# A hand-ordered attention and expert kernel: the second matrix's products run a whole tile behind the first's

## The reference

```python
def _attn_ref(q, kv, w_sr):                 # B=2, N=12288, C=128; kv is 384 x 32 per batch
    kv_pool = kv.reshape(B, H // 4, 4, W // 4, 4, C).mean(axis=(2, 4))
    k = v = kv_pool.reshape(B, -1, C) @ w_sr            # 768 keys
    a = softmax(q @ k.T / sqrt(C))
    return a @ v

def _moe_ref(x, w_gate, w1, w2):            # E=8 experts, D=128, F=1024
    e = argmax(x @ w_gate); gate = softmax(x @ w_gate)[e]
    return gate * (relu(x @ w1[e]) @ w2[e])

def _moe2_ref(x, w_gate, w_output_gate, w1, w2):
    # as _moe_ref, and the result is also scaled by sigmoid(x @ w_output_gate)[e]
```

## Time and profile before

| what | value |
|---|---|
| time, median of 3 runs | 1875.98 us (1874.28 to 1877.02) |
| span of the profiled execution, first to last instruction | 2009.7 us |
| busy in that span | PE 1918.1, DVE 1342.6, ACT 1054.8, POOL 739.4 us |
| attention stage in the profile | up to about 640 us |
| layer 1's tiles in the profile | about 640 to 1377 us |
| layer 2's tiles in the profile | about 1377 to 1994 us |

### The profile page before, as it was taken

How to read it: one execution, slowest core, us unless ns; L and a number is a source line. 1 busy time by engine, 2 the same in 40 slices (tenths; PEclk the granted TensorE clock), 3 DMA queues, 4 the chain that set the end, 5 groups by cost and what they waited for, 6 DMA issues and landing times. The chain is left out here.

```text
span 2009.7 us, 53289 instructions
## 1 busy us (share of the span) xinstructions
PE 1918.1 (95%) x15716; PEld 1879.5 (94%) x15716; DVE 1342.6 (67%) x3525; ACT 1054.8 (52%) x2333; POOL 739.4 (37%) x823
## 2 busy tenths in 40 slices
PE   9999999999999999998999989899999999999998
PEld 7999999999999989898898889888999999999998
DVE  6788887888887666565566666666655555555555
ACT  3777777777776344344344444343444444444444
POOL 5456643466643323222222222222333333333333
PEclk8999999999999999999999999999999999999999
DMA  8355532355533211111321111142211114141111
GB/s 301 104 169 174 178 102 74 109 172 175 173 114 125 67 49 50 42 46 44 118 92 44 45 48 42 51 135 74 66 44 46 43 42 165 42 163 43 46 44 36
DMA packets 138040, 185.88 MB, mean 92 GB/s; under 512 B 17425, under 2 KB 95380, under 8 KB 134368
## 3 DMA queue, kind: packets, MB, share of 16 engines
q1 hardware_dynamic: 112640, 134.16, 20.9%
q0 software_dynamic: 25312, 50.65, 7.1%
HBM read 98.41 MB, written 87.63 MB: 93 GB/s over the span
## 5 line engine op out<-in xcount | busy, mean ns | idle before, releaser
L1718 DVE SCALAR_TENSOR_TENSOR h_lo<-psum,h_hi 128x512 fp32r<-128x512 f32 x800 | 541.2, 688 | 248.3 <-ACT h_hi L1509 198.4
L1509 ACT ACTIVATE h_hi<-psum 128x512 fp32r<-128x512 f32 x800 | 460.6, 598 | 259.1 <-PE psum L1303 244.9
L1303 PE MATMUL psum<-x_hi,w 128*128 128x256 f32 x1600 | 344.7, 290 | 66.6 <-DVE x_lo L1712 48.7
L413 POOL DMA_INDIRECT y_bucket<-kv_store,place x200 | 194.3, 971 | 542.1 <-DVE place L379 484.5
L1303 PE MATMUL psum<-x_hi,w_split 128*128 128x256 f32 x1600 | 339.6, 287 | 9.2 <-issue 2.8
L997 POOL DMA_INDIRECT out<-rows x200 | 193.9, 970 | 405.0 <-DVE rows L1738 368.5
L1303 PEld LDWEIGHTS psum<-x_hi,w 128*128 128x128 f32 x1600 | 270.2, 192 | 75.5 <-issue 55.2
L1320 PE MATMUL psum<-h_hi,w 128*128 128x256 f32 x1600 | 321.6, 285 | 0.7 <-DVE h_lo L1718 0.7
L413 POOL DMA_INDIRECT x_bucket<-rows,place x192 | 190.0, 990 | 293.2 <-DVE place L379 197.7
L1303 PEld LDWEIGHTS psum<-x_hi,w_split 128*128 128x128 f32 x1600 | 265.5, 189 | 17.4 <-issue 10.5
L1320 PEld LDWEIGHTS psum<-h_hi,w 128*128 128x128 f32 x1600 | 266.4, 195 | 1.3 <-DVE h_lo L1718 1.3
(11 more groups left out here) (177 smaller groups left out, 4385.1 us busy)
## 6 DMA issues: line engine op xcount, KB each, us to landing
w_table<-w_split SPq DMA_DIRECT2D x64, 512.0 KB, 3.5
w_raw<-in_moe_w SPq DMA_DIRECT2D x64, 256.0 KB, 4.1
xr<-x_bucket SPq DMA_DIRECT2D x100, 132.0 KB
xr<-y_bucket SPq DMA_DIRECT2D x100, 132.0 KB
kv_store<-in_kv SPq DMA_DIRECT2D x24, 512.0 KB, 9.3
q_in<-in_q SPq DMA_DIRECT2D x48, 256.0 KB, 2.7
w<-w_table SPq DMA_DIRECT2D x12, 1024.0 KB, 6.8
w_split<-w_table SPq DMA_DIRECT2D x8, 1024.0 KB
```

Of the source, the lines that this page charges most:

```text
L413: nc.gpsimd.indirect_dma_start(r.bucket[:, :], bass.IndirectOffsetOnAxis(r.place[:, g, s:s + 1], 0), r.rows[:, g, s, LG:], None, bounds_ch ...
L1303: ins = nc.tensor.matmul(bank[p][:, m * BLOCK:(m + 1) * BLOCK], layer.w1[c % 2][:, hl, f], x[:, c % 2, :], start=k == 0, stop=k == 2)
L1509: nc.scalar.activation(h_hi[:, p, :], bank[p][:, :], ACT.Relu).then_inc(h_hi_done, 1)
L1718: nc.vector.scalar_tensor_tensor(h_lo[:, p, :], bank[p][:, :], 0.0, h_hi[:, p, :].bitcast(F32), ALU.max, ALU.subtract).then_inc(h_lo_done, 1)
```

## The change

The order inside a tile is written anew on PE, ACT and DVE. On PE it becomes: down 0 of c-1; turn_x of c+1; up 0 of c; down 1 of c-1; rank; up 1; down 2 of c-1; up 2; rows of c-2; down 3 of c-1; up 3. All of `down` runs a tile behind `up`, and the rows and gates' products two tiles behind. `down` alternates between bank 4 and bank 7 by tile, and the routing's small results move from bank 7 to bank 6, which the rows also use; so PE now waits at `ranks` until DVE has read the rows of tile c-3, and at `bank_read` until DVE has read the rank's result. A new small DVE instruction per tile, `keep_tags`, copies the token numbers and gates out of `xr` into `tags`, so SP may refill the slot when that is done. SP asks for x first, then the first matrix of tile c+2, then the second matrix of tile c+1 (before: of tile c+2). The one-time steps of the plan move by one tile.

```diff
-        q_bank, o_bank, rank_bank = bank[5], bank[6], bank[7]
+        q_bank, o_bank = bank[5], bank[6]
+        x_bank, tile_bank = bank[5], bank[6]
+        down_banks = [bank[4], bank[7]]
...
         STEPS = {
             1: ["top", "below", "scaled", "cand", "best", "onehot", "sum", "placed", "den"],
-            2: ["skip", "top", "below", "cand", "best", "onehot", "opened", "open_z", "sum", "eps", "den", "placed"],
+            2: ["skip", "top", "below", "cand", "best", "onehot", "opened", "open_z", "placed", "sum", "eps", "den"],
         }
...
-                    wait(pool, up_done, i - NIT if r.n == 1 else i, HP * UNROLL, HP * (2 * gc + 5) + 2)
+                    wait(pool, up_done, i, HP * UNROLL, HP * (2 * gc + 6) + 2)
...
                     if live(i, c, limit[0], UNROLL):
-                        wait(sp, row_step, i, RS * UNROLL, RS * (c - 3))
+                        wait(sp, tags_done, i, UNROLL, c - 3)
                         load_x(i, c, layer_of(i, c, n)).then_inc(x_in[c % 4], 16)
...
-                        sel = opens(i, c + 2, n)
-                        next_w(i, c + 2, n, sel, 0)
                         next_x(i, c + 3, n)
-                        next_w(i, c + 2, n, sel, 1)
+                        next_w(i, c + 2, n, opens(i, c + 2, n), 0)
+                        next_w(i, c + 1, n, opens(i, c + 1, n), 1)
...
                                 pe.wait_ge(p_lo_done, PAIRS * NBLK)
+                            if at(i, c, 1):
+                                pe.wait_ge(r1.row_step, NBLK)
                             wait(pe, layer.w2_in[c % 2], i, 32, 16 * (c // 2 + 1) - 8 * layer.first)
-                            wait(pe, yT_done, i, UNROLL, c)
+                            wait(pe, yT_done, i, UNROLL, c - 1)
...
+                    if c % 2 and routed(i, n) and live(i, (c - 5) // 2, r2.groups, 2):
+                        rank(pe, r2, i, (c - 5) // 2, True)
+
+                def bank_read(i, c, n):
+
+                    if at(i, c, 0) or at(i, c, 2):
...
+                    if c % 2 and routed(i, n) and live(i, (c - 5) // 2, r2.groups, 2):
+                        ns = len(r2.steps)
+                        wait(pe, r2.route_step, i, 2 * ns, ns * ((c - 5) // 2) + r2.steps.index("placed") + 1)
 
                 def tile_body(i, n):
                     for c in range(UNROLL):
                         if at(i, c, 0):
                             add_pv(NIT, -1, PAIRS - 1, 1)
+                        down(i, c - 1, 0, n)
+                        turn_x(i, c + 1)
                         up(i, c, 0, n)
+                        down(i, c - 1, 1, n)
+                        ranks(i, c, n)
+                        up(i, c, 1, n)
                         down(i, c - 1, 2, n)
+                        up(i, c, 2, n)
+                        bank_read(i, c, n)
+                        tile_rows(i, c - 2, n)
                         down(i, c - 1, 3, n)
-                        up(i, c, 1, n)
-                        up(i, c, 2, n)
-                        ranks(i, c, n)
-                        if at(i, c, 0) or at(i, c, 2):
-                            rank(pe, r1, NIT, c // 2 - 2)
-                        turns(i, c)
-                        tile_rows(i, c - 1, n)
-                        turn_x(i, c + 1)
                         up(i, c, 3, n)
-                        down(i, c, 0, n)
-                        down(i, c, 1, n)
                         if at(i, c, 0):
                             turn_rows(NIT, -1)
...
                             oT_out(NIT, -1)
+                        x_high(i, c + 1)
                         h_high(i, c, 0)
+                        if routed and c % 2:
+                            gate_exp(act, r2, i, (c - 5) // 2)
+                        h_high(i, c, 1)
+                        h_high(i, c, 2)
+                        if routed and c % 2 == 0:
+                            route_exp(act, r2, i, (c - 4) // 2)
                         yT_out(i, c - 1)
-                        if routed and c % 2 == 0:
-                            gate_exp(act, r2, i, (c - 4) // 2)
-                        h_high(i, c, 1)
-                        x_high(i, c + 1)
-                        h_high(i, c, 2)
                         h_high(i, c, 3)
...
+                def keep_tags(i, c):
+
+                    if tile_live(i, c):
+                        wait(dve, x_in[c % 4], i, 16, 16 * (c // 4 + 1))
+                        wait(dve, row_step, i, RS * UNROLL, RS * (c - 3))
+                        nc.vector.tensor_scalar(tags[:, c % 4], xr[:, c % 4, :, ID:GATE + 1].bitcast(I32), 0, None,
+                                                ALU.arith_shift_right).then_inc(tags_done, 1)
...
+                        x_low(i, c + 1)
+                        keep_tags(i, c + 1)
                         h_low(i, c, 0)
                         if tail:
-                            steps(*(["best", "onehot"] if odd else []))
+                            steps(*(["top", "below", "scaled", "cand"] if odd else ["sum", "placed", "den"]))
                         else:
-                            steps(*(["best", "onehot", "opened"] if odd else ["den", "gate"]))
...
+                            steps(*(["placed", "sum", "eps"] if odd else ["skip", "top", "below"]))
                         h_low(i, c, 1)
-                        x_low(i, c + 1)
+                        if tail:
+                            steps(*(["best", "onehot"] if odd else ["gate", "place"]))
+                        else:
+                            steps(*(["den", "gate", "place"] if odd else ["cand", "best", "onehot"]))
                         h_low(i, c, 2)
-                        if tail:
-                            steps(*([] if odd else ["placed", "den"]))
-                        else:
-                            steps(*([] if odd else ["placed"]))
+                        if not tail:
+                            steps(*([] if odd else ["opened", "cum"]))
+                        tile_rows_out(i, c - 2, n)
                         h_low(i, c, 3)
```

More of the change, by code:

```diff
@@ L287, in __init__, with rank @@
                 self.all_out = sem(f"all_out{n}")
-        def rank(pe, r, i, gc):
+        def rank(pe, r, i, gc, tiles):
             g = gc % 2
@@ L296, in rank, with route @@
                 wait(pe, r.row_step, i, r.row_steps * UNROLL, r.row_steps * (2 * gc + 3))
-            nc.tensor.matmul(places_ps, before[:, :], r.onehot[:, g], start=True, stop=False)
-            nc.tensor.matmul(places_ps, ones[:, :], r.upto[:, 1 - g], start=False, stop=False)
-            nc.tensor.matmul(places_ps, ones[:, :], bcast_mid(bucket_base[:, :], GSUB), start=False,
+            into = places_ps(tiles)
+            nc.tensor.matmul(into, before[:, :], r.onehot[:, g], start=True, stop=False)
+            nc.tensor.matmul(into, ones[:, :], r.upto[:, 1 - g], start=False, stop=False)
+            nc.tensor.matmul(into, ones[:, :], bcast_mid(bucket_base[:, :], GSUB), start=False,
                              stop=True).then_inc(r.rank_done, 1)
-        def route(dve, r, i, gc, name):
+        def route(dve, r, i, gc, name, tiles):
             if not live(i, gc, r.groups, 2):
@@ L442, in count @@
                 pe.wait_ge(r.route_step, len(r.steps) * (groups - 1) + r.steps.index("placed") + 1)
-                nc.tensor.matmul(counts_ps, ones[:, :], r.total[:, groups % 2], start=True, stop=True) \
+                nc.tensor.matmul(counts_ps(late or self.early_tiles), ones[:, :], r.total[:, groups % 2], start=True, stop=True) \
                     .then_inc(self.counted, 1)
@@ L1502, in x_high @@
                         wait(act, up_done, i, HP * UNROLL, HP * (c - 1))
-                        nc.scalar.activation(x_hi[:, c % 2, :], bank[5][:, 0:BLOCK], ACT.Copy).then_inc(x_hi_done, 1)
+                        nc.scalar.activation(x_hi[:, c % 2, :], x_bank[:, 0:BLOCK], ACT.Copy).then_inc(x_hi_done, 1)
                 def h_high(i, c, p):
@@ L1785, in tile_body @@
                         else:
-                            steps(*(["cum", "open_z"] if odd else []))
+                            steps(*([] if odd else ["open_z"]))
                         early_plan(plan2, 2, i, c)
```

183 lines of the change are left out of this document (101 added, 82 removed).

## The result

The changed kernel takes 1908.19 us (four runs, 1906.71 to 1909.93) where the kernel before takes 1875.38: ratio 1.0177, 95% interval 1.0165 to 1.0189, so it is 33 us slower. The forecast was 1869 us and faster. Its profiled execution took 1908.95 us, as long as its other runs, unlike that of the kernel before.

What follows compares the result with a forecast made beforehand. The prediction took PE to bound the kernel, by its work and its waits. Its terms, -6 - 2 - 4 - 1 + 6 = -7 us on the median, gave 1869 us, with a range of 8 in 10 from 1842 to 1886.

Steps and rivals of the forecast that it cites:

- the counted floor: PE's work in all stages: 6.25 us per tile in layer 1, 5.89 in layer 2, 1870 us in total.
- The choice on which the forecast stood: Profiled execution without idle time and clock loss is 1910.6 us, 34.6 above the median, so timed runs lack most waits.
- the late word is real: Rival, chance 0.14: timed runs partly have layer 1's waits too; 1839 us with half of 74.4 us, 1802 with all.
- The turn a tile ahead: PE's turn of the next x gets a tile of room, covering ACT's late copy: -6 us, bounds 0 and 74.4.
- Down a tile behind: PE's down needs an `h_lo` started a tile ago, so layer 2's 4.2 us of idle time go: -2 us.
- the change of layer: Between the expert layers, a tile of slack mostly covers 6.4 us of PE's idle time: -4 us.
- first tiles: At 640 to 785 us, with 11.2 us of PE's idle time: -1 us.
- the shared bank: PE waits ahead of the rows for DVE to read the rank's result: 0 by cover, 25 us without it.
- the scatters: POOL's four scatters in a row become two and two, making the late word shorter in the profile: no term.
- The matrix loads: Second matrix asked for later, so PE waits about 3 us per bunch, three and a half bunches: +6 us, bounds 0 and +30.
- second matrix comes late: Rival, chance 0.28: PE stands at down 0; six loads late by 3 us give 1894 us, 1881 with the sum's gains.
- What the profile after would show: Span near 1945 us, PE over 98% busy in layer 1, clock 1.00, layer 2 period 5.9 to 6.0 us, idle before down 0.

Runs made afterwards that it cites:

- before_no_loads: The kernel before with no matrix loaded at a change of expert: 1871.3 us, ratio 0.9982.
- before_again: The kernel before, unchanged, profiled once more on a chip where it takes 1990 us: profiled execution 1992.6 us, seven plain runs 1982 to 1993 us.
- before_turn_early: The kernel before with only the next tile's turn and its copies moved to the head of the tile: 1904.7 us against 1990.1 there.
- after_fifth: The changed kernel as it is, on a chip where the kernel before takes 1995.4 us: 1916.7 us, ratio 0.962.
- after_no_loads: The changed kernel with no matrix loaded at a change of expert: 1886.1 us, ratio 1.0059.
- turn_early_no_loads: The kernel before with only the early turn, and no matrix loaded at a change of expert: 1883.8 us.
- by_rows_no_loads: The changed kernel with its turn back behind the rows transposes, and no matrix loaded at a change of expert: 1883.1 us.
- two_ahead_tags: The kernel before, turning the tile two ahead in the old place, copies at the next tile's head, tags kept, x asked for first: 1876.4 us, ratio 1.0002.
- after: The changed kernel as it is, first measurement: 1908.19 us, ratio 1.0177; profiled execution 1908.95 us.
- w2_first: The changed kernel with SP asking for the second matrix ahead of the first: 1897.5 us, ratio 1.0119.

## Why the prediction failed

*What bounds the kernel, and the counted floor.* Right for the 1875 chips: 6.25 and 5.89 us per tile were counted, 6.28 and 5.90 measured, and the floor of 1870 us is before_no_loads' 1871.3. So the old kernel had next to no waits to give there but 3.7 us of loads. (The kernel before with its loads has no profile from such a chip; its times say it.)

*The choice on which the forecast stood* (the timed runs can't have most of these waits): right for the runs it was made for, wrong in its reason. Most likely the profile and the median were of two kinds of chip. Which chip that profile ran on isn't known, but its waits are those of before_again, whose plain runs were as long. On the 1990 chips plain runs have the waits too, and the change takes them out: 79 us. The rival "the late word is real" (0.14) describes those chips, if with 1802 to 1839 us on the wrong base: it took the waits off the median of a chip that had none. The 34.6 us that spoke against it weren't PE's work: in part they were waits that "busy" hides. A matmul is shown 0.28 us long and starts every 0.113, so a gap of up to 0.17 us behind it isn't idle. By the starts such hidden gaps sum to 27 us in the two expert layers of the profile before, where the clock is full, and to 0.4 us in before_no_loads. Another 7 us are the attention stage's: the first matmul of up starts at 647.2 us there and at 639.9 in before_no_loads.

*The sum.* Forecast: -6 - 2 - 4 - 1 + 6 = -7 us. Measured: +12.5 for the early turn, +18.4 for the loads, +2.3 for all the rest, which is +33.2. So the sum failed at two of its terms.

*The turn a tile ahead, -6.* The step that failed by sign. On the 1875 chips nothing waited for the copy, so its room was worth nothing, and setting the turn apart from the rows transposes costs 12.5 us. The forecast counted the transposes as moved, at the same price; the trace before held only one group per tile, so nothing in it showed what a second one does to the matmuls behind it. That cost was in none of the bounds. For the 1990 chips the forecast's mechanism (a tile of room covers the late word) is borne out in before_turn_early; in after_fifth the word is no longer late.

*Down a tile behind, -2, the change of layer, -4, first tiles, -1.* No gain of these is seen: after_no_loads is above before_no_loads, and its one wait at the change of layer is 1.5 us, as there. The 2.3 us of loss left over fit the spacing behind the rank's products.

*keep_tags, the shared bank, the scatters, 0.* Right as to waits: no idle piece ahead of the rows, DVE 72% busy.

*The matrix loads, +6.* The term that was mis-sized: +18.4 on balance. The mechanism, the place and the wait were as written, about 3 us ahead of down 0, at four bunches where three and a half were counted. Two things were left out. The clock behind the wait was not priced: of the 22.1 us, 13.3 are idle pieces (15.0 less the 1.7 that after_no_loads has too), and the 17 us at 1.2 GHz behind the four waits cost another 8.5. And the wait was netted down to 2 us for costs that the old kernel has in all only 3.7 us of. The Trainium skill (TensorE: Matmul & The Clock Gate, HAM oscillation — how this bites in real kernels) describes a kernel in which waits for DMAs let TensorE's clock fall to 1.2 GHz, so that the work behind each wait starts there. The trace agrees, with 0.56 behind 2.72 us of idle time.

*The rival "second matrix comes late"* (0.28, 1881 to 1894) named the larger half: 1875.4 + 18.4 is 1894, its upper end. The other 14.8 us no rival had.

*What the profile after would show:* PE over 98% busy in layer 1, clock 1.00, the pieces ahead of down 0: right. A span near 1945: 1907, which is of a chip of the other kind than the profile before, as it seems, and so no test of that forecast. Layer 2's period of 5.9 to 6.0: 5.99 apart from the loads, and that it was the upper end was the sign of the loss.

Not settled: why a group of two transposes is followed by the slow spacing and why it lasts 28 matmuls in one tile and 4 in the next. Behind a group that ends with the turn, the first step between wide matmuls is 0.205 to 0.208 us where the fast spacing follows at once, and 0.199 to 0.203 where 2, 4, 28 or 46 slow steps do, in six traces (before_no_loads, after_no_loads, turn_early_no_loads, by_rows_no_loads, two_ahead_tags and after). So it may be a matter of phase at restart; no run changed that phase alone. Why on 1990 chips some words come up to 3 us late isn't known either, nor whether two_ahead_tags gains there.

## What to carry to other kernels

Ask of a profile whether it and the median come from the same chip: a span 7% above the median most likely meant a different chip here, and the same change was worth 4% on one kind and cost 2% on the other. Where PE is the bound, count matmuls per microsecond and not only idle time, since an engine that never waits can still get slower. In this kernel keeping PE's short products in one group kept it fast. Two transfers that are asked for together need room for both. And a wait costs more than its length where the clock falls behind it: those of 2.7 to 3.4 us cost 4.4 to 6.8 us here.

## What the runs showed of the hardware

Matmuls of 256 columns at the full clock follow each other in about 0.1133 or about 0.1178 us. Which of the two is decided behind a group of transposes or narrow products, and then holds for a run of matmuls. The Trainium skill (TensorE: Matmul & The Clock Gate, Back-to-back issue gap) has 0.109 us for 256 columns by its formula, which it gives for an isolated matmul; for streams with weight loads, as this one is, it says that the spacing is another and gives none for 256 columns. No step in the expert layers of any trace here is as short as 0.109. The prediction applied the formula without that reservation; nothing in its sum rests on it.

Behind waits of 2.7 to 3.4 us the granted clock fell to 1.2 GHz in the changed kernel, and so it did in the profile before, behind waits of 1.9 us; in w2_first it stayed at 2.4 GHz behind waits of 1.4 to 2.0 us.

Two kinds of chip, or of states that last as long as a batch, run the same program in 1875 and 1990 us. On the first (before_no_loads) the copy behind the turn starts 0.04 us after the turn's end in all 76 tiles from 785 to 1265 us; on the second (before_again) it starts over 1 us after it in 32 of 66, and up to 2.9 us.
